# Attention taken two duos at a time on TensorE, with two low parts of w1 and the expert turns placed elsewhere

## The chip, the cores and the metric

The kernel runs on one core of a Trainium2 chip. The metric is the device time of one launch in microseconds. Before the change three runs gave 628.32 (median), 628.30 and 629.27.

## What is computed

There are three stages in a row, all in float32.

```python
# attention: q, k, v are [2, 8, 768, 64]; a key counts if it is one of the first 4 (sinks)
# or at most 127 positions back
scores = (q @ k.T) / 8
scores = where(is_sink | in_window, scores, -1e9)
a = exp(scores - max(scores)); a = a / (sum(a) + 1e-9)
x = a @ v                                  # -> [1536, 512]
# gated product: w_a, w_b are [512, 1536], w_out is [1536, 512]
y = ((x @ w_a) * (x @ w_b)) @ w_out
# experts: 8 experts of capacity 192; (token, expert) pairs are taken in falling order of logit
logits = y @ w_gate
out[mask_e] = relu(y[mask_e] @ w1[e]) @ w2[e]   # w1[e] is [512, 1024], w2[e] is [1024, 512]
```

## The kernel before

The program is written engine by engine, and each engine works through its queue in the order in which the loops issue it; semaphores tie the queues together.

**Attention.** Heads are handled in 8 pairs, and queries in 6 tiles of 128. A *unit* `u` is one head and one tile; a *duo* `g` holds the two heads of a pair for one tile, so there are 48 duos (`DUOS`) and 6 per pair (`QT`). Tile 0 sees 128 keys, tile 1 sees 256, the other four see 256 and the 4 sinks (`keys`). For a duo, TensorE computes the scores of both units (`scores`, L1167), VectorE adds the mask and takes the maximum (`mask`, L824), ScalarE takes the exponential with its row sums (L674), VectorE forms the reciprocals (L868, L871), GpSimd (L546) and VectorE (`probabilities`, L833) scale one head each, TensorE turns the probabilities (`turn`: the sinks in L1181, the blocks of 128 in L1187), ScalarE copies the turned blocks out of PSUM (L682) and VectorE the turned sinks (L862), TensorE multiplies with the values (`values`, L1228, and L1233 for the sinks), and ScalarE and VectorE write the high and the low part of x (L637, L848). A float32 number is carried as a high and a low part of the faster type wherever its product needs both.

The order of the work is written by hand. TensorE's loop over `g` issues scores of duo `g`, turns of duo `g - 3` and values of duo `g - 4`; after the last scores, halves of the gated product are put between the rest (`gated_half`). VectorE's loop issues two masks of duo `g`, the copy of the sinks of duo `g - 3`, the low part of x of duo `g - 5`, then reciprocals and probabilities of duo `g - 1`. ScalarE's issues the high part of x, two exponentials and one copy of turned blocks, and in some rounds a piece of the first columns of w_a and w_b (`HIGH_AT`); GpSimd takes the low parts of these pieces (`LOW_AT`). The eight PSUM banks are three for scores (`SB_`), two for turned blocks, two for x, and one, `TB`, for turned sinks.

SyncE's queue issues the loads in program order, all of them in one DMA queue: q and k of a pair wait until the scores of the pair two before are done (L357, L358), v of a pair until its values are done (L366, with two small loads of the sinks' rows in L368). Behind v of pair 3 stands `woT`, the turned w_out (L448), and behind that q and k of pair 4:

```python
for p in range(2, PAIRS):
    load_qk(p)      # waits s_ready, UPP * (p - 1)
    load_v(p)       # waits pv_done, QT * (p - 1)
    if p == 3:
        sp.dma_start(woT[:, :, :], w_outT).then_inc(woT_in, 16)
```

**Gated product and routing.** 48 steps follow, each with 24 products of 384 columns (L1241 to L1243), then the products with w_out and, between them, the choice of tokens, which ends in the lists `idx` (L1076).

**Experts.** GpSimd gathers the rows of each expert by an indirect DMA in two halves (`gather`, L581). TensorE turns them (`expert_in`, L1448), multiplies with w1 in 8 column blocks (`expert`, L1466 and L1468) and then with w2 (`out_rest`, L1489, and `out_first`). w1 is split by ScalarE (L723) and VectorE (`low_w1`, L1054), w2 by ScalarE (L766) and GpSimd (L600). Before the first expert TensorE runs wide filler products (`keep_clock_up_wide`, L1143). SyncE issues w2 and w1 of expert 1 after both gathers 0 and 1 have landed (L408, L409).

The functions that the change touches, with the line numbers of the profile:

Of the kernel before, what the change touches and what calls it, by code (L numbers as in the profile page):

```python
# [16 lines left out]
def build(nc, qT, kT, v, w_a, w_b, w_out, w_outT, w_gate, w1, w2, out, y_dram, l_dram, n_sink, window):  # L17
# [11 lines left out]
    DUOS = UNITS // 2  # L29
    KD = DM // P  # L30
# [22 lines left out]
    KEPT_UP = [4, 4, 4, 3]  # L53
# [18 lines left out]
    HIGH_AT = {5 * j + 10: divmod(j, PIECES) for j in range(2 * PIECES)}  # L72
    LOW_AT = {5 * j + 12: divmod(j, PIECES) for j in range(2 * PIECES)}
    assert max(LOW_AT) < DUOS
    assert window == P and D == 64 and NF % FG == 0 and E <= TILE and S % P == 0 and S % C == 0 and N % CY == 0 and N < BIG and REST == P // 2

    def sinks_before(g):

        return (g // QT) * (QT - 2) + max(0, g % QT - 2)
# [52 lines left out]
    with ExitStack() as ctx:  # L132
# [72 lines left out]
        pe_sb = [sb(f"pe_sb{i}", [P, MID], F32, att) for i in range(6)]  # L205
        pn_sb = [sb(f"pn_sb{i}", [P, MID, 2], F32, att) for i in range(4)]
        pT_sb = [sb(f"pT_sb{i}", [P, 4 * P], F32, att) for i in range(2)]

        sinkT_sb = [sb(f"sinkT_sb{i}", [P, P], F32, att) for i in range(2)]
# [113 lines left out]
        w2h_done, w2l_done = sem("w2h_done"), sem("w2l_done")  # L323
        yg_in = [[sem(f"yg_in{i}{h}") for h in ("first", "rest")] for i in range(2)]
# [8 lines left out]
        SB_, PT_, OB_, TB = banks[0:3], banks[3:5], banks[5:7], banks[7]  # L333
# [140 lines left out]
        def _(pool):  # L474
# [10 lines left out]
            for i in range(2):  # L485
                pool.memset(sinkT_sb[i][:, :], 0.0).then_inc(sinkT_cleared, 1)
# [52 lines left out]
            for g in range(DUOS):  # L539
# [3 lines left out]
                pool.wait_ge(inv_ready, g + 1)  # L543
                if g >= 4:
                    pool.wait_ge(pT_ready, g - 3)
                pool.tensor_scalar(pn_sb[g % 4][:, 0:w, h], pe_sb[(2 * g + h) % 6][:, 0:w], inv[:, 2 * g + h:2 * g + h + 1],  # L546
                                   None, ALU.mult).then_inc(pn_ready[h], 1)
                if g in LOW_AT:
                    low_ab_piece(*LOW_AT[g])

# [53 lines left out]
            gather(0)  # L604
            gather(1)
# [19 lines left out]
        def _(act):  # L625
# [38 lines left out]
            for g in range(DUOS + 5):  # L664
                if g >= 5:
                    x_high(g - 5)
                if g < DUOS:
                    _, n, ns = keys(g % QT)
                    w = n * P + ns
                    for u in (2 * g, 2 * g + 1):  # L670
                        act.wait_ge(s_masked, u + 1)
                        if g >= 3:
                            act.wait_ge(pn_ready[u % 2], g - 2)
                        act.activation(pe_sb[u % 6][:, 0:w], s_sb[u % 4][:, 0:w], ACT.Exp, bias=nmx[:, u:u + 1],  # L674
                                       scale=-1.0, accum_out=rowsum[:, u:u + 1]).then_inc(exp_done, 1)
# [877 lines left out]
```

## Time and profile before

| | |
|---|---|
| median of three runs | 628.32 us |
| the profiled execution, its own time | 630.48 us |
| its span, from first to last instruction | 628.8 us |
| TensorE busy | 613.8 us, 98% |
| VectorE, GpSimd, ScalarE busy | 423.0, 318.9, 291.8 us |
| mean granted TensorE clock | 0.996 |
| moved by DMA | 94.37 MB, mean 150 GB/s |

Times in the rows are in us from the start of the span. A row of a timeline gives the start, the time from the start of its first to the end of its last instruction, the engine, the line, the operation with what it writes and reads, and in brackets how long the engine had been idle and what released it. Matmuls overlap, so the spacing of their starts says what they cost, and their durations do not. A float32 matmul leaves two records. PE is TensorE, DVE is VectorE, ACT is ScalarE, POOL is GpSimd, SPq is SyncE's queue of DMA issues.

### The profile page before, as it was taken

Reading aid. Unit: us, or ns where it says so; the run is one execution under the profiler, and the core shown is the slowest. Engines: PE = TensorE matmul, PEld = TensorE weight load, DVE = VectorE, ACT = ScalarE, POOL = GpSimd, SP = SyncE. Lnnn points to the kernel's source line nnn. Section 1 sums busy time; section 2 is a strip of 40 time slices with the busy share of each in tenths; the row PEclk is TensorE's granted clock in tenths of the full one; section 3 lists DMA queues with packets and bytes.
Section 4 is the critical chain, followed back from the end, with each engine's and each line's share of the span. In section 5 each row is a group of like instructions: output and inputs, shape, how many; then the busy total and the mean of one; then the engine's idle time right before and its main releaser. Section 6 shows DMA issues by size and latency. Waiting matters only on the chain.

```text
span 628.8 us, 13301 instructions
## 1 busy us (share of the span) xinstructions
PE 613.8 (98%) x4722; PEld 508.0 (81%) x4722; DVE 423.0 (67%) x1416; ACT 291.8 (46%) x695; POOL 318.9 (51%) x230
## 2 busy tenths in 40 slices
PE   8999999999999999999999999999898999999995
PEld 6666668999899899989987787777676888888894
DVE  5888883111146519989898998888955577676670
ACT  6899893333333333332332224243535656666541
POOL 7566563554455645545456651000094766668741
PEclk9999999999999999999999999999999899999999
DMA  9374232333473464346214151414459478866600
GB/s 284 99 283 151 78 94 66 104 101 100 122 215 111 124 202 134 115 145 179 68 34 142 60 186 35 152 51 119 168 208 388 133 230 298 295 236 238 204 25 26
DMA packets 76097, 94.37 MB, mean 150 GB/s; under 512 B 4448, under 2 KB 53888, under 8 KB 75392
## 3 DMA queue, kind: packets, MB, share of 16 engines
q1 hardware_dynamic: 73696, 86.82, 42.6%
q0 software_dynamic: 2048, 6.29, 3.1%
q8 instruction: 39, 0.64, 0.4%
q10 hardware_dynamic: 288, 0.41, 0.2%
q14 instruction: 26, 0.21, 0.1%
HBM read 87.16 MB, written 6.34 MB: 149 GB/s over the span
## 4 chain that ended last, share of the span: by engine, by line
PE 93%; DVE 4%; issue 1%; DMA 0%; POOL 0%; ACT 0%; POOLq 0%; DVEq 0%
PE bank L1241 14%; PE bank L1364 14%; PE bank L1243 13%; PE bank L1242 13%; PE bank L1466 9%; PE bank L1167 4%; PE bank L1228 4%; PE bank L1489 4%; PE bank L1187 4%; PE bank L1468 4%; PE bank L1254 2%; PE bank L1408 1%; PE bank L1315 1%; PE bank L1233 1%; PE bank L1448 1%
## 5 line engine op out<-in xcount | busy, mean ns | idle before, releaser
L530 POOL TENSOR_TENSOR wl_ab<-raw_ab,wh_ab 128x1024 fp32r<-128x1024 f32 x46 | 110.2, 2395 | 111.5 <-ACT wh_ab L643 111.5
L1241 PE MATMUL bank<-xh,wh_ab 128*128 128x384 f32 x384 | 132.1, 344 | 0.0
L1243 PE MATMUL bank<-xh,wl_ab 128*128 128x384 f32 x384 | 128.7, 335 | 0.0
L1242 PE MATMUL bank<-xl,wh_ab 128*128 128x384 f32 x384 | 128.5, 335 | 0.0
L600 POOL TENSOR_TENSOR w2l<-w_raw,w2h 128x1024 fp32r<-128x1024 f32 x32 | 75.6, 2390 | 43.7 <-DVE w1l L1054 43.5
L945 DVE TENSOR_TENSOR hid<-hid,bank 128x384 f32<-128x384 f32 x48 | 26.6, 554 | 98.3 <-ACT hid L657 98.3
L657 ACT ACTIVATE hid<-bank 128x384 f32<-128x384 f32 x48 | 23.6, 492 | 144.6 <-PE bank L1243 144.6
L1241 PEld LDWEIGHTS bank<-xh,wh_ab 128*128 128x128 f32 x384 | 72.0, 188 | 10.1 <-issue 8.3
L1466 PE MATMUL bank<-xg,w1h 128*128 128x384 f32 x256 | 77.3, 369 | 2.8 <-issue 2.6
L1242 PEld LDWEIGHTS bank<-xl,wh_ab 128*128 128x128 f32 x384 | 72.2, 188 | 0.0
L1243 PEld LDWEIGHTS bank<-xh,wl_ab 128*128 128x128 f32 x384 | 72.1, 188 | 0.0
L546 POOL TENSOR_SCALAR pn_sb<-pe_sb,inv 128x260 f32<-128x260 f32 (+2 forms) x48 | 50.4, 1051 | 33.2 <-DVE inv L871 33.1
L1468 PE MATMUL bank<-xg,w1l 128*128 128x192 f32 x256 | 64.8, 253 | 0.0
L915 DVE TENSOR_SCALAR_CACHE_REDUCE ge<-lb,L 128x768 bf16<-128x768 f32 (+1 forms) x48 | 58.1, 1209 | 1.2 <-PE bank L1254 1.1
L581 POOL DMA_INDIRECT yg<-y_rows,idx x16 | 16.9, 1056 | 77.3 <-DVE idx L1076 73.6
L1466 PEld LDWEIGHTS bank<-xg,w1h 128*128 128x128 f32 x256 | 48.9, 191 | 5.2 <-issue 3.3
L674 ACT ACTIVATE pe_sb<-s_sb,nmx 128x260 f32<-128x260 f32 (+2 forms) x96 | 46.5, 485 | 12.9 <-DVE nmx L824 12.7
L1468 PEld LDWEIGHTS bank<-xg,w1l 128*128 128x128 f32 x256 | 49.8, 195 | 0.2
L707 ACT ACTIVATE wh_out<-raw_out 128x512 fp32r<-128x512 f32 x24 | 15.1, 632 | 73.3 <-PE bank L1364 73.3
L1090 DVE TENSOR_REDUCE bank<-bank 128x128 f32<-128x256 f32 x64 | 27.7, 433 | 31.8 <-PE bank L1468 29.0
L643 ACT ACTIVATE wh_ab<-raw_ab 128x1024 fp32r<-128x1024 f32 x46 | 48.4, 1052 | 0.0
L1054 DVE TENSOR_TENSOR w1l<-w_sb,w1h 128x1024 fp32r<-128x1024 f32 x32 | 37.7, 1217 | 10.7 <-ACT w1h L723 7.3
(162 smaller groups left out, 1274.3 us busy)
## 6 DMA issues: line engine op xcount, KB each, us to landing
w_sb<-in_moe_w_dram SPq DMA_DIRECT2D x8, 2048.0 KB, 10.3
w_raw<-in_moe_w_dram SPq DMA_DIRECT2D x32, 512.0 KB, 8.5
raw_ab<-in_moe_w_a_dram SPq DMA_DIRECT2D x48, 256.0 KB, 3.1
raw_ab<-in_moe_w_b_dram SPq DMA_DIRECT2D x48, 256.0 KB, 3.5
raw_out<-in_moe_w_out_dram SPq DMA_DIRECT2D x24, 256.0 KB, 2.7
lb<-logit_rows SPq DMA_DIRECT2D x4, 1536.0 KB, 6.6
v_sb<-in_v_dram SPq DMA_DIRECT2D x8, 384.0 KB
woT<-in_moe_w_outT_dram SPq DMA_DIRECT2D x1, 3072.0 KB, 10.7
```

The source lines that it names most:

```text
L530: pool.tensor_tensor(wl_ab[s % 2][:, :], raw_ab[s % 3][:, :], wh_ab[s % 2][:, :].bitcast(F32), ALU.subtract).then_inc(abl_done, 1)
L546: pool.tensor_scalar(pn_sb[g % 4][:, 0:w, h], pe_sb[(2 * g + h) % 6][:, 0:w], inv[:, 2 * g + h:2 * g + h + 1], None, ALU.mult).then_inc(pn ...
L600: pool.tensor_tensor(w2l[e % 2][:, at, :], w2_raw[e % 2][:, at, :], w2h[e % 2][:, at, :].bitcast(F32), ALU.subtract).then_inc(w2l_done, 1)
L643: act.activation(wh_ab[s % 2][:, :], raw_ab[s % 3][:, :], ACT.Copy).then_inc(abh_done, 1)
L674: act.activation(pe_sb[u % 6][:, 0:w], s_sb[u % 4][:, 0:w], ACT.Exp, bias=nmx[:, u:u + 1], scale=-1.0, accum_out=rowsum[:, u:u + 1]).then_ ...
L915: dve.tensor_scalar(earlier, lb[:, 0:c, e, :], li, 0.0, ALU.is_ge, ALU.add, accum_out=rank_parts[:, t, e, 0:1]).then_inc(ge_ready, 1)
L1241: pe.matmul(dst, lh, rh, start=first, stop=False)
L1242: pe.matmul(dst, lh, rl, start=False, stop=False)
L1243: return pe.matmul(dst, ll, rh, start=False, stop=last)
L1364: mm = pe.matmul(YB_[t][:, :], (yhl if part == 2 else yhh)[z % 2][:, t * P:(t + 1) * P], (wl_out if part == 1 else wh_out)[z % 2][:, :], s ...
L1466: pe.matmul(H2_[m % 4][:, 0:2 * CAP], w1h[:, kk, at], xg[:, kk, :], start=(kk == 0), stop=(kk == KD - 1), skip_group_check=True)
L1468: mm = pe.matmul(H2_[m % 4][:, 0:CAP], w1l[e % 2][:, kk, at], xg[:, kk, 0:CAP], start=False, stop=(kk == KD - 1), skip_group_check=True)
```

## The change

Attention goes by *quads* `q` of two duos (`QUADS` = 24, `QPP` = 3 per pair). TensorE issues the scores of the four units of quad `q`, the turns of the two duos of quad `q - 2`, the turns of their sinks (`turn_sinks`, which come last now), and the values of the two duos of quad `q - 3`. Scores have four banks instead of three; the turned sinks get no bank of their own but free columns of score banks 1 and 3 (`SINKS`), so a turn of sinks waits for the masks of the scores that were just put into that bank, and odd units wait for the copies of sinks. There are eight buffers of exponentials instead of six, and four of turned blocks and of turned sinks instead of two. VectorE computes the reciprocals of four units in one instruction and does it first in a round, puts the low parts of x between the masks, and copies the sinks last. Pieces of w_a and w_b are spread over quads 5 to 20. At the end of attention there are three rounds with a half of the gated product instead of four, and the fourth half follows them.

In the experts, the last two low parts of expert 0's w1 on VectorE wait for `gather_issued`, which a small memset on GpSimd sets after gather 0; the second no longer waits for the first gathered rows. The wide filler has 2 + 3 products instead of 2 + 4. The turns of expert `e + 1` come after the last column block of expert `e` instead of before it.

```diff
-    KEPT_UP = [4, 4, 4, 3]
+    KEPT_UP = [8, 6, 6]
-    HIGH_AT = {5 * j + 10: divmod(j, PIECES) for j in range(2 * PIECES)}
-    LOW_AT = {5 * j + 12: divmod(j, PIECES) for j in range(2 * PIECES)}
+    HIGH_AT = {2 * j + 5: divmod(j, PIECES) for j in range(2 * PIECES)}
+    LOW_AT = {2 * j + 6: divmod(j, PIECES) for j in range(2 * PIECES)}
...
-        SB_, PT_, OB_, TB = banks[0:3], banks[3:5], banks[5:7], banks[7]
+        SB_, PT_, OB_ = banks[0:4], banks[4:6], banks[6:8]
+        SINKS = [SB_[i][0:2 * n_sink, MID:MID + P] for i in (1, 3)]
...
             gather(0)
+            pool.memset(ge_rest[:, 0:1], 0.0).then_inc(gather_issued, 1)
             gather(1)
...
+            for q in range(QUADS + 4):
+                if q >= 4:
+                    x_high(2 * q - 8)
+                    x_high(2 * q - 7)
+                if q < QUADS:
+                    exps(2 * q)
+                    exps(2 * q + 1)
+                if 0 <= q - 2 < QUADS:
+                    pT_copy(2 * q - 4)
+                    pT_copy(2 * q - 3)
+                if q in HIGH_AT:
+                    split_ab_piece(*HIGH_AT[q])
...
+            for q in range(QUADS + 4):
+                if 0 <= q - 1 < QUADS:
+                    reciprocals(q - 1)
+                if q < QUADS:
+                    mask(4 * q)
+                    mask(4 * q + 1)
+                if q >= 4:
+                    x_low(2 * q - 8)
+                    x_low(2 * q - 7)
+                if q < QUADS:
+                    mask(4 * q + 2)
+                    mask(4 * q + 3)
+                if 0 <= q - 1 < QUADS:
+                    probabilities(2 * q - 2, 1)
+                    probabilities(2 * q - 1, 1)
+                if 0 <= q - 2 < QUADS:
+                    sink_copy(q - 2)
...
+            dve.wait_ge(gather_issued, 1)
             low_w1(0, 2)
-            dve.wait_ge(yg_in[0][0], 16)
             low_w1(0, 3)
...
-                if u >= 3:
-                    pe.wait_ge(s_masked, u - 2)
+                if u >= 4:
+                    pe.wait_ge(s_masked, u - 3)
+                if u % 2 == 1:
+                    pe.wait_ge(sinkT_out, sinks_before(max(0, u // 4 - 2)))
...
+            def turn_sinks(q):
+
+                if q % QPP == 0:
+                    return
+                pe.wait_ge(sinkT_out, sinks_before(q))
+                for a in range(2):
+                    pe.wait_ge(s_masked, min(4 * (q + 2) + 2 * a + 2, UNITS))
+                    pe.transpose(SINKS[a], pn_sb[(2 * q + a) % 4][:, P:P + n_sink, :].rearrange("p k h -> p (k h)"),
+                                 ident[:, :]).then_inc(sinkT_ready, 1)
...
-            for g in range(DUOS + 4):
-                if g < DUOS:
-                    scores(2 * g)
-                    scores(2 * g + 1)
-                if g < len(KEPT_UP):
-                    keep_clock_up(PT_[1], KEPT_UP[g])
-                if 0 <= g - 3 < DUOS:
-                    turn(g - 3)
-                if 0 <= g - 4 < DUOS:
-                    values(g - 4)
-                if g >= DUOS:
+            for q in range(QUADS + 3):
+                if q < QUADS:
+                    for u in range(4 * q, 4 * q + 4):
+                        scores(u)
+                if q < len(KEPT_UP):
+                    keep_clock_up(PT_[1], KEPT_UP[q])
+                if 0 <= q - 2 < QUADS:
+                    turn(2 * q - 4)
+                    turn(2 * q - 3)
+                    turn_sinks(q - 2)
+                if 0 <= q - 3 < QUADS:
+                    values(2 * q - 6)
+                    values(2 * q - 5)
+                if q >= QUADS:
...
-            keep_clock_up_wide(banks[7], 4)
+            keep_clock_up_wide(banks[7], 3)
...
-                    if f == KF - 2 and e + 1 < E:
-                        expert_in(e + 1)
+                if e + 1 < E:
+                    expert_in(e + 1)
```

TensorE's queue inside a pair, before: scores of a duo (`k_sb,q_sb`), turn of its sinks (`8x128`), turns, values, values of sinks.

```order
75 L1167 MATMUL bank<-k_sb,q_sb 64x256 x4
76 L1181 MATMUL bank<-ident,pn_sb 8x128
77 L1187 MATMUL bank<-ident,pn_sb 128x128 x4
78 L1228 MATMUL bank<-pT_sb,v_sb 64x128 x4
79 L1233 MATMUL bank<-sinkT_sb,v_sink 64x128 x2
80 L1167 MATMUL bank<-k_sb,q_sb 64x260 x4
81 L1181 MATMUL bank<-ident,pn_sb 8x128
82 L1187 MATMUL bank<-ident,pn_sb 128x128 x4
83 L1228 MATMUL bank<-pT_sb,v_sb 64x128 x4
84 L1233 MATMUL bank<-sinkT_sb,v_sink 64x128 x2
```

And now, over one quad with full widths and the next:

```order
33 L1196 MATMUL bank<-k_sb,q_sb 64x260 x8
34 L1212 MATMUL bank<-ident,pn_sb 128x128 x8
35 L1222 MATMUL bank<-ident,pn_sb 8x128 x2
36 L1263 MATMUL bank<-pT_sb,v_sb 64x128 x4
37 L1268 MATMUL bank<-sinkT_sb,v_sink 64x128 x2
38 L1263 MATMUL bank<-pT_sb,v_sb 64x128 x4
39 L1268 MATMUL bank<-sinkT_sb,v_sink 64x128 x2
40 L1196 MATMUL bank<-k_sb,q_sb 64x260 x8
41 L1212 MATMUL bank<-ident,pn_sb 128x128 x6
```

Two duos' scores stand in one run of eight, their turns in one run, the sinks behind them, and the values of two duos together.

VectorE's queue in the second quad of a pair, now (L837 is a mask with its maximum, L861 the low part of x, L846 probabilities, L881 the copies of turned sinks, L867 the first step of the next reciprocals):

```order
91 L837 ISA s_sb,nmx<-bank,mask_mid 128x260 [waits exp_done,s_ready]
92 L837 ISA nmx 128x1
93 L861 TENSOR_TENSOR xl<-bank,xh 128x128 [waits xh_done] x2
94 L837 ISA s_sb,nmx<-bank,mask_mid 128x260 [waits exp_done,s_ready]
95 L837 ISA nmx 128x1
96 L837 ISA s_sb,nmx<-bank,mask_mid 128x260 [waits exp_done,s_ready]
97 L837 ISA nmx 128x1
98 L846 TENSOR_SCALAR pn_sb<-pe_sb,inv 128x128 [waits pT_ready,inv_ready]
99 L846 TENSOR_SCALAR pn_sb<-pe_sb,inv 128x256 [waits pT_ready,inv_ready]
100 L881 COPY sinkT_sb<-bank 8x128 [waits pv_done,sinkT_ready] x2
101 L867 TENSOR_SCALAR rowsum_eps<-rowsum 128x4 [waits exp_done]
```

Before, the copy of a duo's sinks came right behind its two masks, and each duo had its own two steps to the reciprocals; now the copies come last in a round, behind four masks, two low parts and two probabilities.

The third place is SyncE's queue around pair 3 and 4. It is the same before and after, and what changes is when its waits end.

```order
22 L370 DMA v_sb<-in_v_dram 128x768 [waits pv_done]
23 L372 DMA v_sink<-in_v_dram 4x64 x2
24 L452 DMA woT<-in_moe_w_outT_dram 128x6144
25 L361 DMA q_sb<-in_q_dram 128x768 [waits s_ready]
26 L362 DMA k_sb<-in_k_dram 128x792
27 L370 DMA v_sb<-in_v_dram 128x768 [waits pv_done]
```

The first row waits for 12 duos' values, which TensorE issues at the end of round 15 of duos before and at the end of round 8 of quads now.

## Rows read from the trace of the kernel before

**Rows 1.** The page, part 4: shares of the chain that ended last, by engine.

```profile
PE 93%; DVE 4%; issue 1%; DMA 0%; POOL 0%; ACT 0%; POOLq 0%; DVEq 0%
```

**Rows 2.** Timeline of TensorE: first scores of duo 0, of pair 3 and pair 4.

```profile
4.76 0.71 PE L1167 MATMUL bank<-k_sb,q_sb 64*64 64x128 f32 x8
...
36.97 0.45 PE L1167 MATMUL bank<-k_sb,q_sb 64*64 64x128 f32 x8
...
48.35 0.45 PE L1167 MATMUL bank<-k_sb,q_sb 64*64 64x128 f32 x8
```

**Rows 3.** Timeline of TensorE, one duo of full width and what stands around it.

```profile
51.48 0.66 PE L1228 MATMUL bank<-pT_sb,v_sb 128*64 128x128 f32 x8
51.97 0.39 PE L1233 MATMUL bank<-sinkT_sb,v_sink 128*64 128x128 f32 x4
52.29 0.67 PE L1167 MATMUL bank<-k_sb,q_sb 64*64 64x260 f32 x8
52.89 0.27 PE L1181 MATMUL bank<-ident,pn_sb 128*8 128x128 f32 x1
53.00 0.64 PE L1187 MATMUL bank<-ident,pn_sb 128*128 128x128 f32 x4
53.57 0.66 PE L1228 MATMUL bank<-pT_sb,v_sb 128*64 128x128 f32 x8
```

**Rows 4.** Timeline of VectorE for the same duo: mask, copy of sinks, low part, probabilities.

```profile
52.99 0.43 DVE L824 CUSTOM_DVE_ANT_0 s_sb<-bank,mask_mid 128x260 f32<-128x260 f32 x1 [0.32 <-PE bank L1167]
...
53.70 0.27 DVE L862 COPY sinkT_sb<-bank 8x128 f32<-8x128 f32 x1
53.90 0.27 DVE L848 TENSOR_TENSOR xl<-bank,xh 128x128 fp32r<-128x128 f32 x1
...
54.48 0.36 DVE L833 TENSOR_SCALAR pn_sb<-pe_sb,inv 128x256 f32<-128x256 f32 x1
```

**Rows 5.** Timeline of ScalarE: an exponential, and the next duo's first one.

```profile
57.90 0.50 ACT L674 ACTIVATE pe_sb<-s_sb,nmx 128x260 f32<-128x260 f32 x1
...
59.04 0.51 ACT L674 ACTIVATE pe_sb<-s_sb,nmx 128x260 f32<-128x260 f32 x1
```

**Rows 6.** Timeline of SyncE's issues, and landing times of all loads of k.

```profile
33.57 0.33 SPq L366 DMA_DIRECT2D v_sb<-in_v_dram  x1
...
35.21 0.44 SPq L448 DMA_DIRECT2D woT<-in_moe_w_outT_dram  x1
...
36.23 0.43 SPq L358 DMA_DIRECT2D k_sb<-in_k_dram  x1
...
DMA to landing us min/median/max: 2.9/4.1/11.7
```

**Rows 7.** Timeline of TensorE: the first product of step 2, behind the drain.

```profile
108.69 0.33 PE L1241 MATMUL bank<-xh,wh_ab 128*128 128x384 f32 x1
```

**Rows 8.** Timelines of VectorE and GpSimd at the first gathers.

```profile
454.88 1.21 DVE L1054 TENSOR_TENSOR w1l<-w_sb,w1h 128x1024 fp32r<-128x1024 f32 x1
...
455.13 2.03 POOL L581 DMA_INDIRECT yg<-y_rows,idx  x1 [73.62 <-DVE idx L1076]
457.45 0.93 POOL L581 DMA_INDIRECT yg<-y_rows,idx  x1 [0.30 <-issue]
...
461.51 9.45 POOL L600 TENSOR_TENSOR w2l<-w_raw,w2h 128x1024 fp32r<-128x1024 f32 x4
```

**Rows 9.** SyncE's first load of expert 1, and ScalarE's wait for its w1.

```profile
463.45 2.40 SPq L416 DMA_DIRECT2D w_raw<-in_moe_w_dram  x4
...
479.83 3.90 ACT L723 ACTIVATE w1h<-w_sb 128x1024 fp32r<-128x1024 f32 x4 [3.11 <-DMA w_sb<-in_moe_w_dram]
```

**Rows 10.** Busy time by stretch: length, then PE, PEld, DVE, ACT, POOL, granted clock, DMA.

```profile
483.00:487.38 4.38, 1.94 (x11) 1.56 (x12) 3.71 (x6) 1.21 (x2) 0.96 (x1) 1.00 1.05 386
487.38:490.79 3.41, 3.41 (x15) 3.41 (x14) 1.21 (x6) 1.72 (x5) 3.41 (x2) 0.50 0.17 61
490.79:494.00 3.21, 3.21 (x24) 3.21 (x24) 2.43 (x9) 1.56 (x6) 2.73 (x4) 1.00 0.19 41
```

More of the change, by code:

```diff
@@ L29, in build @@
     DUOS = UNITS // 2
+    QUADS = DUOS // 2
+    QPP = QT // 2
     KD = DM // P
@@ L484, in _ @@
                 pool.memset(v_sink[i][:, :, :], 0.0).then_inc(v_sink_cleared, 1)
-            for i in range(2):
+            for i in range(4):
                 pool.memset(sinkT_sb[i][:, :], 0.0).then_inc(sinkT_cleared, 1)
@@ new lines, in reciprocals, with sink_copy @@
+            def reciprocals(q):
+                of = slice(4 * q, 4 * q + 4)
+                dve.wait_ge(exp_done, 4 * q + 4)
+                dve.tensor_scalar(rowsum_eps[:, of], rowsum[:, of], 1e-9, None, ALU.add).then_inc(eps_done, 1)
+                dve.wait_ge(eps_done, q + 1)
+                dve.reciprocal(inv[:, of], rowsum_eps[:, of]).then_inc(inv_ready, 1)
+            def sink_copy(q):
+                if q % QPP == 0:
+                    return
+                if q < QPP:
+                    dve.wait_ge(sinkT_cleared, 4)
+                for a in range(2):
+                    g = 2 * q + a
+                    dve.wait_ge(sinkT_ready, sinks_before(q) + a + 1)
+                    if g >= 4:
+                        dve.wait_ge(pv_done, g - 3)
+                    dve.tensor_copy(sinkT_sb[g % 4][0:2 * n_sink, :], SINKS[a]).then_inc(sinkT_out, 1)
@@ L1166, in scores @@
                 for half in range(2):
-                    mm = pe.matmul(SB_[u % 3][half * D:(half + 1) * D, 0:n * P + ns],
+                    mm = pe.matmul(SB_[u % 4][half * D:(half + 1) * D, 0:n * P + ns],
                                    q_sb[par][rows, i * P + half * D:i * P + (half + 1) * D], seen,
@@ L1188, in turn @@
                 mm.then_inc(pT_ready, 1)
+            def turn_sinks(q):
+                if q % QPP == 0:
+                    return
+                pe.wait_ge(sinkT_out, sinks_before(q))
+                for a in range(2):
+                    pe.wait_ge(s_masked, min(4 * (q + 2) + 2 * a + 2, UNITS))
+                    pe.transpose(SINKS[a], pn_sb[(2 * q + a) % 4][:, P:P + n_sink, :].rearrange("p k h -> p (k h)"),
+                                 ident[:, :]).then_inc(sinkT_ready, 1)
             def gate_rows(i):
```

110 lines of the change are left out of this document (40 added, 70 removed).

## The prediction

> **What bounds the kernel now.** I read the chain of waits first. It runs through TensorE for 93% of the span [rows 1]. So a change pays where it takes time out of TensorE's queue, and costs where it makes that queue wait. The score matmuls came next: the first starts at 4.76, pair 3 begins at 36.97 and pair 4 at 48.35 [rows 2]. Six duos take 11.38 us, and the eight pairs make a stage of some 90 us. Then TensorE's timeline of one duo [rows 3]: 8 score records from 52.29 to 52.89 (0.60), the turn of the sinks 0.11, four turns 0.57, values 0.49, values of the sinks 0.32. Together that is 2.08 us, and nothing in it waits for another engine.
>
> The neighbours are close behind. VectorE needs 0.35 per mask (two from 52.99 to 53.70), 0.20 for a copy of sinks and as much for a low part of x, 0.38 for the two steps to the reciprocals, and 0.36 for its probabilities [rows 4]. ScalarE needs 0.50 per exponential, and 1.14 for one exponential with the copy of turned rows and the high part of x (57.90 to 59.04), which is 1.64 per duo [rows 5]. A first mask starts 0.70 after the first score of its duo (52.29 to 52.99).
>
> **TensorE's own work.** A run of one kind costs more than its matmuls. Four turns at a spacing of 0.12 would be 0.48, and they hold the queue for 0.57; the last four value records at 0.11 per two would be 0.22, and they hold it for 0.32; the scores' 0.60 holds two passes, which start about 0.27 apart [rows 3]. I put the starts and ends of the three runs at 0.40 per duo. Two duos together pay them once: 0.40 less per quad (bounds 0.25 and 0.45), 1.2 per pair. Without any new wait a pair would take 11.38 - 1.2 = 10.2 us.
>
> **The new waits.** The sinks of a duo are now turned into columns of a score bank, so the second one waits until the fourth mask of the quad whose scores have just been issued is done. VectorE's order is two masks, two low parts of x, two masks. Counted from the quad's first score: 0.70, then 4 x 0.35 and 2 x 0.20, and about 0.1 until it is seen, gives 2.6. TensorE gets there after 1.0 of scores, 0.95 of turns and 0.1, which is 2.05. So it waits 0.55 in the quad whose scores and turns are all full width (4.25 instead of 3.7). The quad with the narrow scores loses about 0.15, since its masks are narrower. The third kind of quad turns no sinks and takes 3.2 to 3.3. A pair then takes 10.2 + 0.55 + 0.15 = 10.9 us (bounds 10.2 with no wait seen, 11.4 if the copies of sinks, which the next scores wait for, come last on VectorE). ScalarE with 2 x 1.64 = 3.3 and a piece of w_a and w_b stays under TensorE's 3.6 on average.
>
> **The start.** The fill is a loop through three engines: masks of a quad, its four exponentials, reciprocals, and only then the masks of the next quad. That is 0.45 for the first mask, 4 x 0.50, 0.38 and 0.2 of hand-overs, about 3.0 us a quad. The first masks come at 4.76 + 0.7, some 5.5, so those of quad 3 start at 14.5 and end at 15.7; only then can the first sinks be turned, and after the first values quad 4 starts near 16.7. Quad 6 (pair 2) follows at 24.1 and quad 9 (pair 3) at 24.1 + 10.9 = 35.0, where the old order has 36.97: 2 us gained by here.
>
> **The transfer that comes late.** SyncE issues v of pair 3 once the values of pair 1 are done, at 33.57; behind it in program order stand woT (3 MB, 35.21) and q and k of pair 4 (36.23), and this k lands 11.7 us after its issue, the longest of all loads of k, at 47.93 [rows 6]. TensorE needs it at 48.35 [rows 2]: 0.4 to spare. From v's issue to k's landing it is 14.4 us. The old order has eight duos of TensorE's work in that time, because values trail scores by four duos. The new order has values trail by three quads, and v of pair 3 goes out when quad 9 starts. Only three quads, 10.9 us, lie between that and the scores of pair 4. So TensorE waits at quad 12 until 35.0 + 0.1 + 14.4 = 49.5, about 3.6 us, with turns and values queued behind the scores, and is then 1.1 **later** than the old order. Every gain up to here is lost. SyncE's order is as before, so nothing moves that load. The loads of the other pairs have no 3 MB ahead of them and need under 8 of the 10.9 us.
>
> Four pairs remain: 49.5 + 4 x 10.9 = 93.1 for the end of the scores, where the old order has 48.35 + 4 x 11.38 = 93.9. The drain has the same work in both (turns, values, four halves of gated products): 14.8 us before, up to 108.69 [rows 7], and 14.75 by my sum of the new one. The stage ends near 107.8, 0.9 earlier.
>
> **The clock.** In the span one stretch has half the granted clock (1.2 in place of 2.4 GHz): 487.38 to 490.79, right after 4.38 us in which TensorE was busy for 1.94 [rows 10]. Full speed gives 24 records in 3.21 us, this stretch 15 in 3.41, so a stretch costs 1.4 us. A wait of 3.6 us at quad 12 leaves TensorE idler than that. I count one such stretch, part of it inside the wait or under the sinks' wait: +0.9 (bounds 0 and 1.7). The Trainium skill (TensorE: Matmul & The Clock Gate, Why this matters for your kernels) says the same of idle gaps between bursts; the trace agrees with its [rows 10].
>
> **The experts.** VectorE's third low part of w1 starts at 454.88 and runs under the first gather's issue, which takes 2.03 us against 0.93 for the second [rows 8]: 1.1 us lost. It now waits until both issues of gather 0 are through, so expert 0's rows come 1.1 earlier; the filler, one wide matmul shorter, follows, and expert 0 starts 0.9 earlier. But both low parts (2 x 1.21) now lie over the two issues of gather 1, in place of one. SyncE loads w2 and w1 of expert 1 only once gather 1 has landed (463.45), and this w1 is what ScalarE waits for until 479.83 [rows 9]; expert 1 has TensorE waiting behind it. The issues of gather 1, over at 461.51, should end 0.2 to 0.9 later: +0.5, and expert 0's 0.9 only lengthens a wait. The block shown by [rows 8] is what the sum goes by. By the Trainium skill (SBUF — State Buffer, Who interferes with whom) whichever instruction issues first holds the shared ports for its whole length; GpSimd could then slip in between the two low parts, which would give the 0.2 and not the 0.9.
>
> Moving the rows of the next expert behind the last column block leaves a kind of run out at six boundaries; at the 0.1 per switch of [rows 3] this is 0 to -0.6: -0.3. The two fillers' count and the larger buffers cost nothing: TensorE waits there anyway.
>
> **Sum**, against the profiled span of 628.8 (that execution took 630.48 outside): -0.9 + 0.9 + 0.5 - 0.3 = +0.2. I carry this to the median of the runs, 628.32, and forecast **628.5 us**, no change. About 0.2% (1.26 us) is what a measurement of this kernel can tell from none.
>
> **Rivals.** *The waits of the sinks are not seen* (masks end sooner than I add up, or TensorE's runs are shorter still). At 10.2 a pair quad 9 starts at 33.8, pair 4 at 48.3, the stage ends at 48.3 + 40.8 + 14.75 = 103.9, 4.8 earlier; with the clock and the experts 624.6. For it: VectorE idles 0.3 us per duo now. Against it: the order of its queue. A half of this, 10.55 a pair, gives 626.6, already faster. *The load of pair 4 is not late*: then 3.6 and 0.9 of clock come back, 624.0. Against it stands a queue that took 14.4 us.
>
> *The clock stays down.* This ends slower. After the wait at quad 12, or in the fill, where TensorE waits for masks in quads 2 to 4, the half clock holds for more than one stretch. Each further one is 1.4 us: one gives 629.9, two 631.3, and one decides. For it: after the fill and after the wait a third of TensorE's records are turns with pauses between; against it: full clock all through the old stage, with the same kinds of work. The Trainium skill (TensorE: Matmul & The Clock Gate, Part 4: PE-mode transpose) has it that a transpose does not count as busy, by which the clock would come back late here; no row of this case bears on that alone.
>
> **How the numbers follow.** No change, with the late load eating what the longer runs give: 0.37. Faster (shorter waits of the sinks, or no late load): 0.37. Slower (clock, or copies of sinks last on VectorE): 0.26. The range takes in most of the first rival and one to two further stretches: 624.8 to 631.0.
>
> **What would show it.** Right: scores of pair 4 start near 49.5, behind k's landing, with over 3 us of idle TensorE; the second turn of sinks follows the fourth mask; one stretch of half clock behind 50; the stage's last product near 108; w1 of expert 1 awaited until about 480.3 less the shift. Wrong: scores of pair 4 at 46, or a pair at 10.2, or half clock over several stretches.

## The result, and the profile after the change

The changed kernel takes **632.01 us** (median of 7 runs, 629.87 to 632.57) where the kernel before, measured beside it, takes 629.14 (7 runs, 628.30 to 630.43): ratio 1.0035, 95% interval 1.0018 to 1.0051. Measured once more (after_again) it took 631.64 against 629.23, ratio 1.0039 (1.0026 to 1.0052). It is slower. The profiled execution of after took 630.23 (span 628.4), that of before 630.48 (span 628.8). They are the low end of after and the high end of before, so their difference doesn't show the 2.9 us, and I compare them stage by stage.

The chain of waits of after, by engine (answers to [rows 1]):

```profile
PE 84%; DVE 5%; issue 4%; DMA 2%; ACT 2%; POOL 2%; SPq 0%; DVEq 0%; POOLq 0%; ACTq 0%
...
PE bank L1276 14%; PE bank L1403 14%; PE bank L1278 13%; PE bank L1277 13%; PE bank L1505 8%; PE bank L1528 4%; PE bank L1507 4%; PE bank L1263 2%; DMA q_sb<-in_q_dram 2%; PE bank L1196 2%; PE bank L1289 2%; PE bank L1212 2%; ACT pe_sb L676 1%; PE bank L1447 1%; PE bank L1354 1%
```

DMA is new in it, with a load of q and k. The timeline of TensorE of after shows where: pair 3, pair 4, and the first product of step 2 (answers to [rows 2, 7]).

```profile
35.10 0.88 PE L1196 MATMUL bank<-k_sb,q_sb 64*64 64x128 f32 x16
...
49.97 1.78 PE L1196 MATMUL bank<-k_sb,q_sb 64*64 64x128 f32 x16 [3.66 <-issue]
51.68 1.98 PE L1212 MATMUL bank<-ident,pn_sb 128*128 128x128 f32 x8
53.45 0.63 PE L1222 MATMUL bank<-ident,pn_sb 128*8 128x128 f32 x2
...
112.25 0.33 PE L1276 MATMUL bank<-xh,wh_ab 128*128 128x384 f32 x1
```

Pair 3 starts 1.87 earlier than before, pair 4 1.62 later after 3.66 of idle TensorE, and step 2 3.56 later. The y products (+3.62) and the first count of the experts' rows (+3.64) keep this difference. SyncE's issues of after, and the landing times of SyncE's loads of k, answer to [rows 6]:

```profile
35.22 0.33 SPq L370 DMA_DIRECT2D v_sb<-in_v_dram  x1
35.59 1.23 SPq L372 DMA_DIRECT2D v_sink<-in_v_dram  x2
36.85 0.44 SPq L452 DMA_DIRECT2D woT<-in_moe_w_outT_dram  x1
37.34 0.43 SPq L361 DMA_DIRECT2D q_sb<-in_q_dram  x1
37.81 0.48 SPq L362 DMA_DIRECT2D k_sb<-in_k_dram  x1
...
DMA to landing us min/median/max: 4.1/5.3/12.1
```

The k issued at 37.81, right behind 3 MB of woT, is read as the one with the longest time, 12.1: it lands at 49.9, and TensorE goes on at 49.97. (Its row calls the idle time "issue", so the load as its cause is shown by the run a_woT_last, not by this row.) Behind the wait, busy time by stretch (columns as in [rows 10]):

```profile
45.00:48.95 3.95, 1.31 (x24) 1.07 (x20) 1.29 (x8) 2.59 (x11) 1.86 (x2) 1.00 0.93 373
48.95:52.36 3.41, 2.39 (x19) 1.67 (x20) 1.66 (x11) 1.22 (x5) 0.00 (x0) 0.50 0.76 275
52.36:55.78 3.42, 3.42 (x25) 2.57 (x27) 1.25 (x6) 2.28 (x8) 0.99 (x2) 0.50 0.02 5
55.78:59.20 3.42, 3.14 (x40) 2.17 (x37) 2.87 (x15) 2.52 (x10) 1.23 (x2) 1.00 0.00 0
```

The granted clock is 0.50 in two stretches, not one. Pair 4 takes 13.36 us, pairs 5 and 6 11.14 and 11.19. Last, GpSimd's gathers and ScalarE's wait for w1 of expert 1 in after (answers to [rows 8, 9]):

```profile
458.77 1.20 POOL L585 DMA_INDIRECT yg<-y_rows,idx  x1 [73.62 <-DVE idx L1103]
460.26 0.93 POOL L585 DMA_INDIRECT yg<-y_rows,idx  x1 [0.30 <-issue]
461.19 0.12 POOL L609 MEMSET ge_rest<- 128x1 bf16 x1
461.50 1.90 POOL L585 DMA_INDIRECT yg<-y_rows,idx  x1 [0.19 <-issue]
463.70 0.92 POOL L585 DMA_INDIRECT yg<-y_rows,idx  x1 [0.30 <-issue]
...
482.73 3.91 ACT L736 ACTIVATE w1h<-w_sb 128x1024 fp32r<-128x1024 f32 x4 [2.47 <-DMA w_sb<-in_moe_w_dram]
```

The four issues take 5.85 from the first start to the last end, where before took 6.37. Of the two issues of gather 1 only the first is long; VectorE's two low parts run from 461.34 to 463.70, and the second issue starts at their end.

### The profile page after: what moved, and what is told of

It reads as the page before. It is cut to its first block, busy times and chain, and to the rows that moved or that the text cites. A ratio compares the mean times of both kernels' runs of the same rounds, so it can differ in the third digit from the quotient of the medians.

```text
span 628.4 us, 13288 instructions
## 1 busy us (share of the span) xinstructions
PE 608.6 (97%) x4725; PEld 511.8 (81%) x4725; DVE 415.4 (66%) x1368; ACT 292.6 (47%) x695; POOL 312.1 (50%) x233
## 4 chain that ended last, share of the span: by engine, by line
PE 84%; DVE 5%; issue 4%; DMA 2%; ACT 2%; POOL 2%; SPq 0%; DVEq 0%; POOLq 0%; ACTq 0%
PE bank L1276 14%; PE bank L1403 14%; PE bank L1278 13%; PE bank L1277 13%; PE bank L1505 8%; PE bank L1528 4%; PE bank L1507 4%; PE bank L1263 2%; DMA q_sb<-in_q_dram 2%; PE bank L1196 2%; PE bank L1289 2%; PE bank L1212 2%; ACT pe_sb L676 1%; PE bank L1447 1%; PE bank L1354 1%
## 5 line engine op out<-in xcount | busy, mean ns | idle before, releaser
L1505 PE MATMUL bank<-xg,w1h 128*128 128x384 f32 x256 | 73.7, 359 | 1.9 <-issue 1.6
L550 POOL TENSOR_SCALAR pn_sb<-pe_sb,inv 128x260 f32<-128x260 f32 (+2 forms) x48 | 42.7, 906 | 41.9 <-DVE inv L869 41.9
```

The source lines that it names most:

```text
L1505: pe.matmul(H2_[m % 4][:, 0:2 * CAP], w1h[:, kk, at], xg[:, kk, :], start=(kk == 0), stop=(kk == KD - 1), skip_group_check=True)
```

## The experiments

Each was timed beside the kernel before. Columns: median and ratio to before with its interval; start and length of pair 4; start of the gate's first product behind attention; time from the first count of the experts' rows to expert 2; starts of the stretches at half clock in the profiled execution, without the one at the end of the span. All but the medians and ratios are read from the one profiled execution of each.

| run | us | ratio | pair 4 | long | gate | to expert 2 | half clock |
|---|---|---|---|---|---|---|---|
| before | 629.1 | | 48.35 | 11.38 | 112.94 | 53.47 | 487 |
| after | 632.01 | 1.0035 [1.0018, 1.0051] | 49.97 | 13.36 | 116.51 | 50.97 | 49 (two), 459 |
| after_again | 631.64 | 1.0039 [1.0026, 1.0052] | 50.75 | 12.62 | 116.52 | 50.76 | 52, 458 |
| a_woT_last | 624.29 | 0.9931 [0.9909, 0.9953] | 46.43 | 11.18 | 110.79 | 50.70 | 452 (two) |
| b_woT_last | 628.19 | 0.9988 [0.9976, 0.9999] | 48.06 | 11.39 | 112.65 | 51.53 | 456 |
| attn_only | 632.13 | 1.0049 [1.0030, 1.0068] | 50.62 | 12.61 | 116.39 | 51.72 | 52, 458 |
| b_turns_last | 626.83 | 0.9965 [0.9952, 0.9978] | 48.55 | 11.38 | 113.15 | 51.44 | none |
| a_w1_early | 630.00 | 1.0019 [1.0008, 1.0030] | 50.42 | 12.16 | 115.75 | 51.13 | 50 |
| b_gather | 630.01 | 1.0010 [0.9994, 1.0026] | 48.95 | 11.38 | 113.53 | 53.53 | 485 (two) |
| aw_masks_first | 624.19 | 0.9923 [0.9908, 0.9939] | 46.56 | 11.06 | 110.36 | 50.76 | 452 |
| aw_low_first | 632.08 | 1.0048 [1.0031, 1.0065] | 48.70 | 12.06 | 117.29 | 51.00 | 459 (two) |
| after_fill_turns | 627.51 | 0.9983 [0.9974, 0.9992] | 50.62 | 11.16 | 114.95 | 50.41 | 457 |
| after_fill_again | 627.45 | 0.9988 [0.9973, 1.0004] | 50.21 | 11.06 | 114.43 | 50.07 | 457 |
| after_fill_products | 627.44 | 0.9985 [0.9970, 1.0001] | 50.18 | 11.06 | 114.41 | 50.03 | 456 |
| aw_early | 624.59 | 0.9937 [0.9924, 0.9949] | 46.79 | 11.17 | 111.13 | 52.80 | 485 |
| aw_clock | 626.20 | 0.9958 [0.9943, 0.9972] | 46.55 | 11.19 | 110.90 | 52.78 | 484 |
| aw_clock_both | 624.72 | 0.9931 [0.9914, 0.9947] | 46.53 | 11.17 | 110.87 | 50.68 | none |
| b_fill_e1 | 628.93 | 0.9997 [0.9986, 1.0008] | 48.09 | 11.37 | 112.67 | 51.80 | none |
| after_fill_e1 | 630.49 | 1.0029 [1.0018, 1.0039] | 50.21 | 13.30 | 116.66 | 51.21 | 49 (two), 459 |
| after_fill_both | 628.33 | 0.9994 [0.9982, 1.0006] | 50.25 | 11.05 | 114.48 | 51.11 | 457 |

### The late load

Theory L: k of pair 4 is late behind woT. In both kernels woT moves to the last pair.

```diff
-                if p == 3:
+                if p == PAIRS - 1:
                     sp.dma_start(woT[:, :, :], w_outT).then_inc(woT_in, 16)
```

Changed kernel (a_woT_last):

> The changed kernel with the 3 MB load of woT issued behind v of pair 7 instead of behind v of pair 3. Theory L (the late load of k of pair 4, and the half clock that its wait brings on, are what the change loses): scores of pair 4 start at 35.1 + 11.2 = 46.3 instead of 49.97, no half clock near 50, quads 12 and 13 take 3.5 and 4.3 instead of 5.5 and 4.4; the stage ends 3.7 + 2.2 = 5.9 us earlier, and the kernel takes about 626, faster than the kernel before by 3. Rival C (the clock falls for another reason, turns with pauses between them): half clock appears elsewhere in the stage all the same and the gain is at most 3.7. Rival W (the waits for turned sinks hold the stage): the gain of the load is taken back by later quads and the time stays over 630.

Kernel before (b_woT_last):

> The kernel before with the load of woT moved in the same way, as a control. Its k of pair 4 landed 0.4 us ahead of need, so theory L expects no difference in the stage: scores of pair 4 at 48.35, step 2 at 108.7, time within 0.2% of before. If the load in itself slowed the stage (another cause than the wait), this run gets faster too.

Timelines of TensorE and of SyncE with woT last in the changed kernel:

```profile
46.43 0.88 PE L1196 MATMUL bank<-k_sb,q_sb 64*64 64x128 f32 x16
...
37.05 0.44 SPq L361 DMA_DIRECT2D q_sb<-in_q_dram  x1
37.53 0.43 SPq L362 DMA_DIRECT2D k_sb<-in_k_dram  x1
```

No idle time stands before pair 4, the stage ends 5.7 earlier than in after, and the median falls by 7.7, to 4.6 below its kernel before. The profiled executions (630.23 and 624.26) differ by 6.0, so 1.7 of the 7.7 is not in them; the part on the upper bunch comes back to it. The same edit in the kernel before leaves the stage within 0.3 of where it was. The late load is settled, and this version beats both kernels.

### Which part costs

attn_only keeps the attention and undoes every edit in the experts:

> The changed attention alone: both low parts of w1, the filler and the place of the expert turns as in the kernel before. Theory: the product of step 2 that follows the stage starts 3.6 us later than before, as in the changed kernel; expert periods return to 19.44 from 19.17 us, and the first expert starts 3.6 and not 4.4 later than before; in all 3.6 us over before, 632 to 633, about 1 to 2 us over the changed kernel. Rival: the expert edits gain nothing by themselves, and this time equals that of the changed kernel.

b_turns_last is the kernel before with the turns of the next expert's rows moved:

```diff
-                    if f == KF - 2 and e + 1 < E:
-                        expert_in(e + 1)
+                if e + 1 < E:
+                    expert_in(e + 1)
```

> The kernel before with the turns of the next expert placed behind its last column block, and nothing else. Theory: each expert from the third on takes 0.27 us less (19.17 instead of 19.44), so 1.4 to 1.9 us in all: 627.3 or so. Rival (my forecast's term): at most 0.1 per boundary, 0.3 in all, no difference in the time.

Attention alone costs 0.49%. Its expert 0 starts 5.0 later than before and not 3.6, with a stretch of half clock at 458. The turns alone give 0.35%. The first w1 products of experts 3 and 4, from TensorE's timelines, before:

```profile
526.06 0.33 PE L1466 MATMUL bank<-xg,w1h 128*128 128x384 f32 x1
...
545.50 0.33 PE L1466 MATMUL bank<-xg,w1h 128*128 128x384 f32 x1
```

and with the turns last:

```profile
523.90 0.33 PE L1466 MATMUL bank<-xg,w1h 128*128 128x384 f32 x1
543.08 0.33 PE L1466 MATMUL bank<-xg,w1h 128*128 128x384 f32 x1
```

An expert takes 19.18 (19.17 in after) in place of 19.44, so a run of one kind left out is worth 0.26 to 0.27 here, not 0.05.

### The edit at the gathers

a_w1_early undoes it in the changed kernel; b_gather makes it alone in the kernel before; aw_early undoes it with woT last.

```diff
-            pool.memset(ge_rest[:, 0:1], 0.0).then_inc(gather_issued, 1)
...
-            dve.wait_ge(gather_issued, 1)
...
+            dve.wait_ge(yg_in[0][0], 16)
...
-            keep_clock_up_wide(banks[7], 3)
+            keep_clock_up_wide(banks[7], 4)
```

> The changed kernel with the edit at the gathers undone: the third low part of w1 goes back ahead of the two that wait for the issues of gather 0, and the filler before expert 0 gets its fourth wide matmul back; attention and the place of the turns stay as changed. Theory G (the edit at the gathers costs, because it lets a stretch of half clock fall just ahead of expert 0, as at 458.56 in the profile of after): no such stretch there, issue of gather 0 again 2.0, expert 0 starts within 0.3 of after's, time 630.0 to 631.0, that is 1 to 2 below after's 632.0. Rival H (as I forecast: the first gather's issue is 1.1 later, and what is lost is hidden until w1 of expert 1 lands): same as after within 0.6, 631.5 to 632.6. Rival I (the edit gains what its 1.1 says): 633.0 or more.

> The kernel before with only the edit at the gathers (third low part of w1 behind the issues of gather 0, three wide fillers instead of four); attention and turns as before. Theory G: a stretch of half clock appears just ahead of or in expert 0, expert 0 starts no earlier than 462.3, time 1 to 2 above the kernel before: 629.5 to 631. Rival H: within 0.6 of the kernel before, 628.3 to 629.5. Rival I: 1 faster, 627.9 or less. Issue of gather 1 ends at or before 461.5 in all of them, since after showed it 0.5 earlier relative to its stage.

> The changed kernel with woT loaded in the last pair and the edit at the gathers undone (the third low part of w1 ahead of the issues of gather 0, four wide fillers). Theory G (that edit costs through half clock ahead of expert 0, 2.0 between after and the run with it undone): no half clock at 452 to 456, time 622.3 to 623.3, the lowest of all. Rival H (what the two runs differed in was chance of the clock): 624.0 to 624.6 as with woT last alone, with the half clock somewhere between 450 and 490.

The medians speak for G in the first (2.0 below after), are unclear in the second, and for H in the third (624.59 against 624.29). The half clock ahead of expert 0 doesn't need the edit: it also stands at 456 and 458 where the edit is undone or never made (b_woT_last, attn_only). But with the changed attention all ten profiles with the edit and without the five products of aw_clock have it, and only one of three with the edit undone; in b_gather it stands at expert 1. What follows the edit in every profile is ScalarE's w1h of expert 1: with it, it starts 25.03 to 26.05 behind the first count of rows (13 profiles), without it 26.13 to 26.69 (seven). So the edit brings this w1 some 0.8 earlier (means 25.61 and 26.40). Expert 0 starts 8.59 behind the count in b_gather, 9.45 in before, and 10.22 in after, where half clock stands ahead of it. Whether the edit also makes that clock fall more often, as theory G has it, isn't settled by one profile a run: the price that G puts on it is contradicted by aw_early, and the 2.0 between the medians of a_w1_early and after stays open.

### What a quad waits for

With woT last, the order on VectorE is varied: four masks and then two low parts of x (masks first), or two low parts and then four masks.

```diff
                     mask(4 * q)
                     mask(4 * q + 1)
+                    mask(4 * q + 2)
+                    mask(4 * q + 3)
                 if q >= 4:
                     x_low(2 * q - 8)
                     x_low(2 * q - 7)
-                if q < QUADS:
-                    mask(4 * q + 2)
-                    mask(4 * q + 3)
```

> The changed kernel with woT loaded in the last pair (so without the late k), and on VectorE all four masks of a quad ahead of the two low parts of x. Theory M (the second turn of sinks waits for the fourth mask, 0.55 per pair's first quad): that turn comes 0.4 earlier after the quad's first score (2.25 in place of 2.64), and the pair shortens from 11.18 to 10.8, stage end 1.5 to 3 earlier than with woT last alone, time near 622.0. Rival N (TensorE's two duos are as long as they are for another reason: the probabilities and low parts then come late for the values and turns): the wait moves behind the values or to the next scores, pair 11.1 to 11.4, time 624 to 625.5.

> As the run with masks first, but with both low parts of x ahead of all four masks. Theory M: the sinks' turn stays where it is or moves by under 0.1 (the fourth mask still ends after the same work), while the first two masks, and with them the exponentials, come 0.4 later: pair 11.2 to 11.6, time 624.3 to 627. Rival N (what the quad waits for is the low parts, for the turns of x): pair 10.8 to 11.0, time 622.5 to 623.5.

Timeline of TensorE with the order as changed, second turn of sinks in pair 6:

```profile
70.61 0.27 PE L1222 MATMUL bank<-ident,pn_sb 128*8 128x128 f32 x1
71.19 0.27 PE L1222 MATMUL bank<-ident,pn_sb 128*8 128x128 f32 x1 [0.30 <-DVE nmx L837]
```

With masks first, the two quads of pair 3 that turn sinks shrink by 0.28 and 0.30 (3.26 to 2.98, 4.47 to 4.17), and the third grows by 0.59, because its values now wait for the low parts:

```profile
40.79 0.38 PE L1221 MATMUL bank<-ident,pn_sb 128*8 128x128 f32 x2
...
45.10 0.66 PE L1262 MATMUL bank<-pT_sb,v_sb 128*64 128x128 f32 x8 [0.52 <-DVE xl L861]
```

With the low parts first, both turns of sinks wait, and a pair takes 12.06 to 12.61:

```profile
38.69 0.27 PE L1221 MATMUL bank<-ident,pn_sb 128*8 128x128 f32 x1 [0.32 <-DVE nmx L837]
39.34 0.27 PE L1221 MATMUL bank<-ident,pn_sb 128*8 128x128 f32 x1 [0.39 <-DVE nmx L837]
```

So the wait for the masks, set by VectorE's order, is shown. But the numbers of theory M missed twice: with masks first it is rival N's that came true (pair 11.06, 624.19), since the order moves the wait behind the values and the remedy gives only 0.1; with low parts first the pair came out longer than both theories said. In the order as changed the quad without any wait takes 3.41.

### The clock behind the wait

While TensorE waits for k of pair 4, it runs 26 turns of the identity (or 14 products of it) into the bank that the next scores overwrite:

```diff
+                if u == 4 * UPP:
+                    pe.wait_ge(s_masked, u - 3)
+                    keep_clock_up(SB_[0], 26)
```

> The changed kernel, and while TensorE waits for k of pair 4 it turns the identity 26 times into the score bank that the next scores overwrite (26 at 0.12 are 3.1 of the 3.66 idle us; the load comes as late as before). Theory K (the idle time is what drops the clock, and turns keep it as matmuls do): pair 4 starts within 0.2 of 49.97, no half clock behind it, pair 4 takes 11.2 in place of 12.2 to 13.4, gate_rows 1.5 to 2.2 earlier than after's 116.51, time 629.8 to 630.6. Rival T (a turn does not count as busy, the rule of the Trainium skill's page on the clock, TensorE: Matmul & The Clock Gate, Part 4: PE-mode transpose): the clock falls as in after, pair 4 takes 12.2 to 13.4, time as after, 631.6 to 632.6.

> The same with 14 products of the identity in place of the turns (128 columns; a wide one of 512 columns took 0.86, so about 0.21 each, 3.0 us). Theory K and rival T both: no half clock behind the wait, pair 4 takes 11.2, gate_rows near 114.5, time 629.8 to 630.6. If it too shows half clock, the idle time at quad 12 is not what drops it. The difference to the run with turns is what tells K from T.

> The changed kernel with 26 turns of the identity in the wait at quad 12, again, beside the unedited one. Theory K (idle time in front of a clock stretch is all that the filler takes away): pair 4 in 11.2, and 1.5 to 2.5 below the unedited kernel of the same call. If the gap is over 3.5 again (627.5 against 632.0 in different calls), the filler also changes what comes later, and the stretches of both profiles behind 450 must show it.

> The changed kernel once more, unedited, for more executions and a second profile. Theory K (its two bunches of times, 629.9 to 630.5 and 632.0 to 632.6, differ by stretches of half clock): a median of 631.5 to 632.3; in a profile of the upper bunch one or two stretches more than the three of the first profile (or the same number with the attention stage's end 0.5 or more later), and everything else alike. Rival W (the bunches differ in the loads, the stretches do not): the same stretches at the same places, and another start of pair 4 or of an expert.

Busy time of TensorE and granted clock by stretch, unedited (after_again):

```profile
46.00:49.00 3.00, 0.97 (x18) 1.00 0.84 307
49.00:52.03 3.03, 1.28 (x17) 1.00 0.91 289
52.03:55.44 3.41, 3.41 (x21) 0.50 0.24 94
```

and with the turns (after_fill_turns):

```profile
46.00:49.41 3.41, 3.41 (x38) 1.00 0.92 342
49.41:52.82 3.41, 2.42 (x26) 1.00 0.74 260
52.82:56.23 3.41, 3.41 (x42) 1.00 0.03 10
```

The load is as late as in after, but the clock stays up and pair 4 takes 11.05 to 11.16 in four profiles, where five without a filler in this wait show 12.16 to 13.36. Theory K holds, and rival T fell: turns held the clock as well as products did. The medians side by side fall by 4.2 (631.64 to 627.45), more than the 1.5 to 2.5 of theory K, and the profiled executions by 2.9 (629.95 to 627.10): 2.1 at the gate, 0.8 in expert 1. The rest of the 4.2 has no cause shown.

### The clock at the experts, and the upper bunch

Of after's 18 executions 8 lie at 629.87 to 630.81 and 10 at 631.64 to 632.57; both profiles are of the lower bunch. Three edits were tried: five products of the identity (128 columns) ahead of the count of rows (aw_clock); 2, 3, 10 and 4 turns ahead of the four pieces of w1 of expert 1 (after_fill_e1, b_fill_e1); and these turns together with the five products (aw_clock_both) or with the 26 turns ahead of pair 4 (after_fill_both). The five products and the turns at expert 1:

```diff
+            for _ in range(5):
+                pe.matmul(banks[7][:, 0:P], ident[:, :], ident[:, :], start=True, stop=True, skip_group_check=True)
...
+                        if m == KF:
+                            keep_clock_up(H2_[(m + 1) % 4], (2, 3, 10, 4)[kk])
```

> The changed kernel with woT loaded in the last pair, and five products of the identity (128 columns, about 1.1 us in all) in the 1.13 us in which TensorE waits for the first names before the rows' numbers are counted. Theory K (the stretch of half clock at 452 follows from the idle time ahead of it): no half clock between 450 and 460, expert 0 starts 9.3 to 9.7 after the first names' matmul in place of 11.6, time 622.3 to 623.3. Rival D (the routing's gaps are too many for one filler, or the clock falls at expert 1 instead): half clock within 0.5 of where it was or between 470 and 490, time 623.9 to 624.6.

> The changed kernel with woT last, the five products ahead of the first names (they moved the half clock from 452 to 483.79), and the same turns in the wait at expert 1. Theory K: no half clock but at the end, expert 0 at 459.6, expert 1 takes 22.5, time 622.0 to 622.8, and little spread. Rival D (the clock falls at yet another place): 624 to 626 with a stretch between 460 and 510.

> The kernel before, and while TensorE waits for w1 of expert 1 it turns the identity 2, 3, 10 and 4 times into a bank that nobody reads (19 at 0.12 are 2.3 of the 3.0 idle us). Theory K (this wait is where the kernel before loses its clock): no half clock between 480 and 500, expert 1 takes 22.5 to 23.2 in place of 24.25, time 627.0 to 627.9, and the executions at 630 and above gone. Rival D (it falls elsewhere, or only in a few executions): within 0.4 of the kernel before.

> The changed kernel with 2, 3, 10 and 4 turns of the identity in the wait at expert 1 alone; the wait at quad 12 as changed. Theory U (the upper bunch of the changed kernel, 631.6 to 632.6, is made of executions that lose the clock at expert 1 too, at 1.7 to 2.0 each): that bunch is gone, median 629.9 to 630.6. Rival V (the upper bunch comes from the attention stage or from ahead of expert 0, since the filler at quad 12 brought the median down by 4.2 where its profiles show 2.9): two bunches as before, median 631.0 to 632.2.

> Both fillers. Theory U: 627.0 to 627.6 as with the one at quad 12, and its few executions at 630 and above gone. Rival V: a few of 12 at 630 and above again. Under both pair 4 takes 11.2.

aw_clock was a miss (626.20 against the 622.3 to 623.3 of theory K): nothing at 452, expert 0 3.2 earlier, and then a longer wait at expert 1 with the stretch there, as the busy time of TensorE shows:

```profile
480.00:483.79 3.79, 1.21 (x6) 1.00 1.04 391
483.79:487.20 3.41, 3.41 (x14) 0.50 0.69 255
```

With both fillers no stretch is left but at the end, and yet aw_clock_both takes 624.72 and its expert 2 starts at 501.74, where a_woT_last, with two stretches at 452, takes 624.29 and has 501.81. A clock lost ahead of expert 0 is **hidden** by the wait for w1 of expert 1; lost at expert 1 it costs 1.7 (before against b_fill_e1) to 2.1 (aw_clock against aw_clock_both); four profiles have 52.8 to 53.5 to expert 2, the others 50.0 to 51.8. Nor is it lost there each time: in b_turns_last TensorE was busy for 1.36 of 3.41 in this wait, and the clock stayed.

```profile
483.41:486.82 3.41, 1.36 (x7) 1.00 1.05 388
486.82:490.23 3.41, 3.41 (x25) 1.00 0.34 121
```

b_fill_e1 shows no stretch, and its median is that of before, as rival D said. That fits if most executions of before lose nothing there, which no profile shows. after_fill_e1 came out as theory U said (12 executions, 629.74 to 631.29, median 630.49, nothing at 631.6 and above). after_fill_both did not: 5 of 12 at 629.5 to 629.8, and the median 0.9 above that of the filler at quad 12 alone. The mean granted clock of each execution says a little more. In after_fill_both the five have 0.993 to 0.994 and the other seven 0.995 to 0.998, where one stretch at half clock is 0.003 of the span. In after and after_again the upper ten have 0.986 to 0.989 and the lower eight 0.989 to 0.992. So lost clock goes with the longer times, but the ranges touch, and these means don't say where it is lost. What makes the upper bunch is **not settled**. Clock lost at expert 1 fits its size and after_fill_e1, but no profile of it was caught, and after_fill_both speaks against that place.

## Why the prediction was wrong

Forecast 628.5, range 624.8 to 631.0, no change; measured 632.0, slower. The late load was foreseen with its mechanism and its size. What failed is the clock term behind it, +0.9 where the profile shows 2.2, and with it the 10.9 for a pair, which is 11.17. Because of these and of the later start of pair 4 the stage ends 3.5 later than the sum has it. Two more terms of the sum erred the other way, by 2.6 together. Of the 3.5 us of the miss, 0.8 is the base (628.32 was the median of three runs; before has 629.14 beside after), 0.9 these errors, and some 1.7 the upper bunch, whose cause is open.

- **The fill and pair 3**: 35.0 forecast, 35.10 measured. Right, by 24.1 for quad 6 (23.92) and 10.9 for a pair (11.18), whose errors partly cancel.
- **The late load**: pair 4 forecast at 49.5 after 3.6 of idle TensorE; measured 49.97 and 3.66. Right, and shown by a_woT_last. "The load of pair 4 is not late" was given 624.0; without woT ahead of it the kernel takes 624.29. That this is so near is luck: the stage then gains 2.1 against before, not the 4.5 of that rival, and the experts give the rest.
- **The clock**, "I count one such stretch: +0.9": mis-sized. Pair 4 took 13.36, or 2.2 above the 11.17 of its neighbours (in the five profiles without a filler there, 1.0 to 2.2). Two stretches came, and only 1.0 of the first lay in the wait (48.95 to 49.97). The rival "The clock stays down" had this mechanism, with 629.9 for one further stretch. One reason given for it, that turns don't hold the clock, is refuted by the filler: what dropped it is the idle time, since either filler in it kept the clock.
- **10.9 a pair**: 11.17. The wait of the second turn of sinks is where it was put, but the quads of a pair take 3.46, 4.31 and 3.41 with woT last, where the sum had about 3.4, 4.25 and 3.25. The last kind waits for nothing, so the saving by longer runs was put too high; that is argued, not tried.
- **The end of the stage**: step 2's first product at 112.25 against 108.69 - 0.9 + 0.9 = 108.7. The 3.5 between are 0.5 at the start of pair 4, 1.6 in pair 4, 0.5 in pairs 5 and 6, and 0.9 from there through the drain.
- **"The issues of gather 1 should end 0.2 to 0.9 later: +0.5"**: they ended 0.5 earlier relative to the stage, and w1 of expert 1 came 0.7 earlier in after (0.8 in the means above). Only the first issue of gather 1 was held up (1.90). That is the alternative which I named and did not take, that GpSimd slips in between the two low parts, as the Trainium skill has it (SBUF — State Buffer, Who interferes with whom). The trace agrees in so far as the issue ends 0.9 behind the first low part; it doesn't show VectorE held up in turn, since the two low parts took 2.36 together, no more than two of them elsewhere (their mean is 1.22 each). And what gather 0 gained (2.03 to 1.20 for its first issue, where I had 1.1) stands ahead of gather 1 too, which the sum left out. The 0.9 for expert 0 shows in b_gather; in after it was lost to half clock.
- **"At six boundaries: -0.3"**: at 0.27 each -1.6 (the profile shows 1.35 of it over the five periods from expert 2 to expert 7), and -2.1 in the median of b_turns_last. I took the 0.1 of attention's short runs for a switch between products of 384 and 512 columns.

From the profiles the sum becomes +3.6 - 0.8 - 1.6 = +1.2 on some 629.1, which is 630.3: after's lower bunch (its eight executions have a median of 630.23). The further 1.7 of the median is the upper bunch, and stays open.

## What to carry to other kernels

A shorter stage pulls its consumers towards loads that are issued by program order: compute for each load the work that lies between the event that releases it and its use, in the new order, and move the large load that nobody needs yet (here one line, 7.7 us between the medians and 6.0 between the profiled executions). Price a wait of several us on TensorE with the clock that follows it, and if the wait can't go, fill it. Do not fill a gap whose end is hidden: it lengthens the next wait, where the clock can then fall (aw_clock, 1.9 slower than a_woT_last).

## What was unexpected of the hardware

Turns of the identity held the granted clock through a 3.7 us wait as well as products did (pair 4 in 11.05 to 11.16 against 11.06), although the Trainium skill (TensorE: Matmul & The Clock Gate, Part 4: PE-mode transpose) has it that transposes don't count as busy in the same way; no row here agrees with it. Behind nearly the same wait (3.66 to 3.92) the clock fell at 49 for two stretches (after, after_fill_e1) or at 50 to 52 for one (a_w1_early, after_again, attn_only), which cost pair 4 2.2 or 1.0 to 1.5 us; after and after_again are the same program. And an indirect DMA issue on GpSimd took 1.90 beside two back-to-back operations of VectorE of 1.18 each, and the others 0.92 to 1.20 beside none. The 1.90 are the 1.0 that the first operation still had to run and the issue's own 0.9, and not both operations.
